# Where VectorE reads its loop bounds in the second expert layer, and two more blank matmuls ahead of the second head's maxima

## The reference

```python
# stage 1: 2 x 8 heads of 768 x 64; a query sees the keys of its own cluster
q_assign = argmax(q_n @ c_n);  k_assign = argmax(k_n @ c_n)
scores = where(q_assign == k_assign, q @ k.T / 8, -1e9)
x = softmax(scores) @ v
# stage 2 (first layer): 8 experts of 512 -> 1024 -> 512, tokens with x @ w_skip > 0 only
out[do_compute] = x + gate * (relu(x @ w1[e]) @ w2[e])
# stage 3 (second layer): all tokens, each to the expert with its largest gate logit
h = relu(x[mask] @ w1[e])
out[mask] = gate_w * sigmoid(x @ w_output_gate)[:, e] * (h @ w2[e])
```

## Time and profile before

| | us |
|---|---|
| runs of the kernel before | 686.12, 688.14, 689.12 |
| median | 688.14 |
| profiled execution, its own time | 690.86 |
| its span (first to last instruction) | 689.1 |
| TensorE busy in it | 653.1 |
| VectorE busy in it | 441.5 |
| mean granted TensorE clock | 0.989 |

### The profile page before, as it was taken

One profiled execution on the slowest core, in us unless ns is written; L12 is line 12 of the kernel. 1 busy time (PEld: TensorE's weight loads), 2 busy tenths in 40 slices (PEclk: granted clock), 3 DMA queues, 4 the chain that ended last, 5 costly groups with the idle time before them and its releaser, 6 DMA issues.

```text
span 689.1 us, 14698 instructions
## 1 busy us (share of the span) xinstructions
PE 653.1 (95%) x5430; PEld 536.3 (78%) x5440; DVE 441.5 (64%) x869; ACT 393.6 (57%) x586; POOL 291.9 (42%) x288
## 2 busy tenths in 40 slices
PE   9889999999999988999999999888999999899995
PEld 5578888888888876579999998546877778687784
DVE  7868888878888857755455635674357447854721
ACT  5558999999999886240343322414437447553611
POOL 4257999998999962022212311101111211322121
PEclk9999999999999999999999999998999999999998
DMA  9301122111121348748499962743552753961010
GB/s 281 91 1 48 48 70 71 48 48 48 49 79 38 111 160 309 303 140 301 166 318 373 352 227 104 275 180 115 190 211 98 278 190 124 339 231 37 16 50 32
DMA packets 46078, 105.90 MB, mean 154 GB/s; under 512 B 5539, under 2 KB 11683, under 8 KB 46016
## 3 DMA queue, kind: packets, MB, share of 16 engines
q1 hardware_dynamic: 38464, 87.65, 36.6%
q0 software_dynamic: 4624, 12.70, 5.7%
q10 hardware_dynamic: 2928, 4.72, 2.0%
HBM read 87.64 MB, written 13.37 MB: 147 GB/s over the span
## 4 chain that ended last, share of the span: by engine, by line
PE 38%; DVE 14%; issue 3%; DVEq 2%; DMA 2%; ACT 1%; ACTq 0%; POOL 0%; POOLq 0%
PE hT_ps_layer L1525 10%; DVE w_rest_layer L1354 5%; DVE w_lo L1243 5%; PE y_ps_layer L1586 3%; PE y_ps_layer L1536 3%; PE y_ps_layer L1540 2%; PE y_ps_layer L1578 2%; PE y_ps_layer L1543 2%; PE hT_ps_layer L1569 2%; PE hT_ps_layer L1563 2%; PE hT_ps_layer L1562 2%; PE y_ps_layer L1583 2%; PE x_turn_layer L1511 1%; PE hT_ps_layer L1462 1%; DMA x<-x_mid 1%
## 5 line engine op out<-in xcount | busy, mean ns | idle before, releaser
L441 POOL TENSOR_TENSOR probs_lo<-probs,probs_hi 128x768 f16<-128x768 f32 x89 | 146.4, 1653 | 35.6 <-ACT probs_hi L356 33.4
L568 DVE TENSOR_REDUCE max_halves<-turn 128x1 f32<-128x384 f32 x180 | 94.8, 553 | 33.2 <-PE turn L732 31.5
L348 ACT ACTIVATE probs<-scores 128x768 f32<-128x768 f32 x96 | 80.0, 833 | 11.3 <-PE scores L760 10.2
L356 ACT ACTIVATE probs_hi<-scores 128x768 f16<-128x768 f32 x96 | 80.3, 836 | 1.2 <-PE pv L784 0.9
L1525 PEld LDWEIGHTS hT_ps_layer<-xT_layer,w 128*128 128x128 f32 x640 | 73.0, 192 | 1.0 <-DVE xT_layer L1347 0.2
L1525 PE MATMUL hT_ps_layer<-xT_layer,w 128*128 128x128 f32 x640 | 73.1, 275 | 0.0
L1173 ACT ACTIVATE w_hi<-w 128x1024 fp32r<-128x1024 f32 x64 | 62.5, 1049 | 16.6 <-issue 13.6
L732 PE MATMUL turn<-kB,qB 96*128 96x384 f32 x180 | 68.6, 402 | 2.0 <-DVE max_halves L568 1.6
L1655 POOL DMA_INDIRECT out_dram<-x,y_token_layer x17 | 17.6, 1038 | 115.6 <-DVE x L1408 115.6
L1178 ACT ACTIVATE hT_hi_layer<-hT_ps_layer 128x512 fp32r<-128x512 f32 x20 | 12.0, 598 | 82.7 <-PE hT_ps_layer L1525 82.7
L760 PE MATMUL scores<-qA,kA 128*128 128x384 f32 x192 | 54.5, 365 | 2.0 <-ACT probs_hi L356 2.0
(11 more groups left out here) (259 smaller groups left out, 1539.8 us busy)
## 6 DMA issues: line engine op xcount, KB each, us to landing
w<-in_moe_w_dram SPq DMA_DIRECT2D x32, 2048.0 KB, 9.3
w<-in_v_dram ACTq DMA_DIRECT2D x4, 768.0 KB, 7.3
qk_raw<-in_q_dram SPq DMA_DIRECT2D x16, 192.0 KB, 3.2
qk_raw<-in_k_dram SPq DMA_DIRECT2D x16, 192.0 KB, 3.1
qB<-qA SPq DMA_DIRECT2D x16, 192.0 KB, 2.7
kB<-kA SPq DMA_DIRECT2D x16, 192.0 KB, 3.2
x_src<-x SPq DMA_DIRECT2D x2, 1536.0 KB, 16.9
x_mid<-x SPq DMA_DIRECT2D x2, 1536.0 KB, 18.3
```

Source lines behind the costliest of these rows:

```text
L348: nc.scalar.activation(probs[slot][:].rearrange("p (n c) -> p n c", n=2), sc[kt % 2][:, :, 0:HALF], ACT.Exp, scale=SCALE).then_inc(probs_r ...
L356: nc.scalar.activation(p_hi[slot][:].rearrange("p (n c) -> p n c", n=2), sc[kt % 2][:, :, 0:HALF], ACT.Exp, scale=SCALE).then_inc(probs_re ...
L441: nc.gpsimd.tensor_tensor(p_lo[slot][:], probs[slot][:], p_hi[slot][:], ALU.subtract).then_inc(p_lo_pool, 1)
L568: nc.vector.tensor_reduce(mh[:, u // 2, u % 2:u % 2 + 1], turn[b][:, 0:HALF], AX.X, ALU.max).then_inc(turn_free[b], 1)
```

## The change

Three things change. First, `WARM_MAXIMUM` goes from 4 to 6. Second, `tiles` reads an expert's two numbers behind the tile loop of the expert before; with `loads_late` they are read behind the hook `after`, without it ahead of `after`. ScalarE in both layers and VectorE in the first layer pass `loads_late=True`, which is the order that they had. TensorE and GpSimd pass nothing and have no hook `after`, so their order stays too. What is left is VectorE in the second layer: its two reads now come ahead of `w1_rest` and `split`. Third, `x_to_lo(0)` and `split(0, 0, 0)` of the second layer move into the hook `lead`, so VectorE reads the first expert's two numbers ahead of them. The hook `before` is now called `between`.

```diff
-    WARM_START, ..., WARM_MAXIMUM = 16, 5, 3, 4, 3, 3, 3, 4, 4
+    WARM_START, ..., WARM_MAXIMUM = 16, 5, 3, 4, 3, 3, 3, 4, 6
...
-    def tiles(eng, body, before=None, after=None, lead=None, numbered=False):
+    def tiles(eng, body, between=None, after=None, lead=None, numbered=False, loads_late=False):
         eng.wait_ge(table_done, 1)
+
+        def at_expert(e):
+            return (eng.value_load(table[0:1, 0, e:e + 1], min_val=1, max_val=NM),
+                    eng.value_load(table[0:1, 1, e:e + 1], min_val=0, max_val=NT_MAX - 1))
+
+        n, base = at_expert(0)
+        if lead is not None:
+            lead()
         for e in range(E):
             pair, par = divmod(e, 2)
-            n = eng.value_load(table[0:1, 0, e:e + 1], min_val=1, max_val=NM)
-            base = eng.value_load(table[0:1, 1, e:e + 1], min_val=0, max_val=NT_MAX - 1)
-            if e == 0 and lead is not None:
-                lead()
-            if before is not None:
-                before(e, pair, par, base)
+            if between is not None:
+                between(e, pair, par, base)
             with eng.Fori(0, n) as j:
...
+            if e + 1 < E and not loads_late:
+                n, base = at_expert(e + 1)
             if after is not None:
                 after(e, pair, par)
+            if e + 1 < E and loads_late:
+                n, base = at_expert(e + 1)
...
-                tiles(act, body, split, after)
+                tiles(act, body, split, after, loads_late=True)
...
-                tiles(act, body_turned, split, w1_split)
+                tiles(act, body_turned, split, w1_split, loads_late=True)
...
-                x_to_lo(0)
-            split(0, 0, 0)
             if first:
+                split(0, 0, 0)
                 dve.wait_ge(gates_turned, 1)
...
+            def first_parts():
+                x_to_lo(0)
+                split(0, 0, 0)
...
-            tiles(dve, body if first else body_turned, after=after, numbered=not first)
+            if first:
+                tiles(dve, body, after=after, loads_late=True)
+            else:
+                tiles(dve, body_turned, after=after, lead=first_parts, numbered=True)
```

More of the change, by code:

```diff
@@ L216, in attention @@
             rest_count[h, kt] = 1 + sum(rest_by_dve(*o) == rest_by_dve(h, kt) for o in rest_count)
-    WARM_START, WARM_CEN, WARM_ASSIGN, WARM_SECOND, WARM_MASKS, WARM_MAX, WARM_SCORES, WARM_TURNED, WARM_MAXIMUM = 16, 5, 3, 4, 3, 3, 3, 4, 4
+    WARM_START, WARM_CEN, WARM_ASSIGN, WARM_SECOND, WARM_MASKS, WARM_MAX, WARM_SCORES, WARM_TURNED, WARM_MAXIMUM = 16, 5, 3, 4, 3, 3, 3, 4, 6
     def wait(eng, s, value):
```

## The result

The changed kernel takes 680.14 us (median of 4 runs, 679.36 to 680.66) against 688.63 us for the kernel before in the same comparison: ratio 0.9882, 95% interval 0.9853 to 0.9910, 8.5 us faster. The forecast was 681.0 us in a range of 677.5 to 684.5. The profiled execution took 680.66 us with a span of 678.9 us, 10.2 us less than the profiled execution before; the forecast for that route was 681.5. One later run of the changed kernel took 718.68 us at a mean granted clock of 0.85, a slower state that no other run here was in; it is in no median and no table.

The account below looks back on a forecast made before the run. TensorE was taken to be held up by VectorE's stream, late through register reads. Profiled route 690.86 - 6.3 (reads) - 1.6 - 1.5 (clock) = 681.5, median route 680.3 with half the clock; forecast 681.0 us, range 677.5 to 684.5.

Parts of the forecast that it names:

- What bounds: Second layer: TensorE waits for VectorE, 7.1 us at L1586 and 1.9 at L1578; register reads make VectorE late.
- Six boundaries, 0.65 us each: Second-layer expert boundaries: reads partly hidden beside L1398 bring y_out 0.65 us earlier each, 3.9 us in all.
- The rule of strict first-in-first-out queues: VectorE's boundary reads: if queue order bound them too, they would stand behind L1398, giving 1.5 us at six boundaries.
- The seventh boundary, 1.03 us: Behind the expert with one tile: reads fit under running instructions, so TensorE's whole 1.03 us stall is gained.
- First expert, 1.34 us: Second layer's start: reads hidden in VectorE's idle time after the gate reduction, 1.34 us gained, TensorE's stall falling to 0.58.
- Clock, second layer, 1.60 us: First expert's w2 part: with 0.58 us idling instead of 1.92 the clock stays up, gaining 1.60 us in the profiled execution.
- Six blanks, 1.5 us: Second head's wait in attention: two more blanks fit into idle time and avert the clock's fall, 1.5 us.
- reads in the queue: Rival at VectorE's boundaries: reads wait behind L1398, 2.8 us plus clock terms, 682 to 685 us; chance 0.14.
- the path moving to ScalarE: Rival: another engine takes over the boundaries, only first expert and clock pay, 2.9 us, about 685.2; chance 0.07.
- the slower case: Rival: reads ahead of L1243 delay low parts past the 2.3 us cover at L1569, 694 us; chance 0.02.
- the one of nothing measurable: Rival: second-layer gains under 3.4 us and clock falls elsewhere, so no measurable difference; chance 0.03.
- What is late next: Second-layer boundaries after the change: VectorE was to remain the late engine, by about 0.3 us.

Follow-up runs that it names:

- first_only: Kernel before with only the first expert's low parts moved behind its register reads, four blanks: 686.50 us, ratio 0.9976.
- bounds_only: Kernel before with only the register reads of experts 1 to 7 moved ahead of the low parts, four blanks: 681.44 us, ratio 0.9916.
- after_again: The changed kernel run once more, nothing altered, beside later kernels on one chip: 680.17 us, ratio 0.9885 to the kernel before.
- blanks_only: Kernel before with six blanks in place of four and nothing else: 688.83 us, ratio 1.0003.
- reads_only: Changed kernel with four blanks in place of six, both moves of the reads kept: 679.72 us, ratio 0.9884 to the kernel before.
- inside_4: reads_inside with four blanks in place of six in the second head's wait: 677.61 us, ratio 0.9833 to the kernel before.
- reads_doubled: Changed kernel with VectorE making every boundary read twice in the second layer: 689.97 us, ratio 1.0018 to the kernel before.
- reads_inside: Changed kernel with VectorE's second-layer reads between issuing w1's four low parts and waiting for them: 676.17 us, ratio 0.9827 to the kernel before.

## Why the prediction was right, point by point

- **What bounds**: right. TensorE's stalls at L1586 and L1578 were the reads' doing; first_only and bounds_only each removed the stall that the step named.
- **Six boundaries, 0.65 us each**: the mechanism was right, the term a little small. The low parts came 0.47 us late, not 0.61, because the read starts 0.15 us behind L1398's start (now L1406) and not 0.3. Gain by the distance from one boundary to the next: 0.72 to 0.83 us each, 4.6 for six against 3.9. The sign named for it was also a little off: 0.8 to 0.9 us of idling ahead of L1243, ending in "issue", was 0.73, put down to ScalarE.
- **The rule of strict first-in-first-out queues** (the Trainium skill, TensorE: Matmul & The Clock Gate, section "Architectural detail: the array is 16× 32×32, not 1× 128×128"), applied to register reads, gave 1.5 us for these boundaries; the measured 4.6 decides against it for them.
- **The seventh boundary, 1.03 us**: right that the stall vanishes whole. From the `y_out` at 585.46 to that at 599.27 stood 13.81 us before, and 12.55 stand now (578.16 to 590.71), 1.26 us less.
- **First expert, 1.34 us**: measured 1.21 at TensorE's product. The low part of the first input (L1361, now L1370) began 3.50 us behind the gate reduction's start where it had been 3.36, which makes up the difference. The reads show no part in that: ScalarE's high part of the input, which it waits for, came 0.14 us later too (2.87 us behind the gate reduction's start, 2.73 before). Both distances lie almost wholly in the third stretch at 0.50; in after_again, without it, the low part comes 2.29 us behind. The prediction overlooked this stretch altogether, and lost nothing by it only because both profiled executions have it.
- **Clock, second layer, 1.60 us**: exactly that in the two profiled executions (7.67 to 6.07). That a stall of 0.6 us keeps the clock up held in all ten profiles that have it. That one of 1.9 us brings it down was too firm: it did in two of three, and bounds_only kept a stall of 1.77 us at the clock of 1.00. Over all runs the clock's part of the gain is about 1 us, against the 1.55 us of half of both falls.
- **Six blanks, 1.5 us**: 1.46 us in the profiled pair, and nothing in the median: blanks_only 1.0003 (0.9985 to 1.0021), four against six on the fastest kernel 0.4 us within its scatter. The step that failed is "Will the fall be averted? I take yes": the fall behind the second head is not a property of four blanks, for the profiled executions of first_only, bounds_only, reads_only and inside_4, all with four, had none there, so there was often nothing to avert. Nor did the idle times that it compared come out: TensorE idled 0.30 us before L746 and not 0.19, as a blank takes 0.21 us and not 0.27, so the two together are 1.41 us, more than the 1.36 given as harmless, and the clock stayed up in executions with 0.73 and 1.11 us, the very 1.84 said to bring it down. Whether six lower its frequency by a little stays open; these runs can't tell 0.4 us.
- **Sum**: 681.0 forecast, 680.14 measured. The reads gave about 7 us at equal clock against 6.3 forecast; the clock gave about 1 us in the median where both falls would have been 3.1. One term was too small and the other too large, so part of the nearness is luck: taken from 688.14 us the forecast was a gain of 7.1 us, and the measured gain, from 688.63, is 8.5.
- **The rivals**: reads in the queue, the path moving to ScalarE, the slower case and the one of nothing measurable all fell. reads_doubled shows how near the slower one lies: 1.26 us of delay was given as the point where the move stops paying, and with 1.22 us more than the change's own 0.47 the kernel stands at 1.0018 of the kernel before.
- **What is late next**: VectorE by 0.3 us, as said; reads_inside took that away, and TensorE then has no wait at a boundary.

## What to carry to other kernels

A read of a loop bound into a register costs an engine's instruction stream 0.6 us whether or not its arithmetic unit is busy, so its place matters: put it where arithmetic has been issued and is still running, ahead of a wait, and it costs nothing (reads_inside); behind a wait for finished writes it costs all of itself (the kernel before). When a stall is read from idle time, add what the break costs beside it: matmuls in a row overlap, and those on both sides of a stop lose that. Here it was 0.27 us for each stop (0.49 less 0.22). And a profile is one execution: a fall of the clock in it is worth its 1.2 to 1.6 us only in that execution, so compare runs of equal mean clock before a part of a change is credited with it.

## What the runs showed of the hardware that was not expected

- VectorE's register read (TENSOR_LOAD, 0.31 us) with its follow-up of 0.21 us runs beside VectorE's own arithmetic, 0.15 us behind the start of the instruction issued just before it.
- A stop of TensorE costs more than its idle row: 0.49 us for 0.22 us of idling at a boundary (reads_inside against the changed kernel).
- Stalls of 1.8 to 1.9 us left the granted clock at 1.00 in one execution (bounds_only) and at 0.50 in others (before, blanks_only).
- Over 49 runs of the kernel before, the time follows the mean granted clock, 686.4 us at 0.997 and 689.3 at 0.991 to 0.992. One stretch of 3.4 us at 0.50 cost 1.21 us between two executions of the changed kernel.
